# Layer 2's output projection in rounded passes, with casts and middle taps done by DMAs

## What is computed

```python
def _moe2_ref(x, w_in, conv_w, w_out):          # x: 4 x 1088 x 128
    h = np.maximum(x @ w_in, 0.0)               # 128 -> 1024 hidden channels
    conv_out = sum(conv_w[k] * hp[:, k:k + S, :] for k in range(3))   # hp is h, padded by one token
    gate = 1.0 / (1.0 + np.exp(-conv_out))
    return (h * gate @ w_out)                   # 1024 -> 128
```

## Time and profile before

| | |
|---|---|
| median of 3 runs | 256.98 us (256.5 to 289.55) |
| profiled execution, its own time | 256.51 us |
| its span, first to last instruction | 254.7 us |
| granted TensorE clock | 1.00 of full |
| instructions | 4283 |

### The profile page before, as it was taken

The page is one execution under the profiler, slowest core; times in us unless marked ns, Lnnn a source line. Parts: engine busy times, 40 slices in busy tenths (PEclk is TensorE's granted clock), DMA queues, the critical chain, the costliest instruction groups (busy, mean ns, idle before and its releaser), DMA issues.

```text
span 254.7 us, 4283 instructions
## 1 busy us (share of the span) xinstructions
PE 247.2 (97%) x1522; PEld 210.7 (83%) x1522; DVE 220.2 (86%) x404; ACT 157.0 (62%) x325; POOL 28.4 (11%) x90
## 2 busy tenths in 40 slices
PE   8999999999999999989999999999999999999995
PEld 7999999998989999978887777778778777777752
DVE  0847888899998688897799999999979999997992
ACT  2351733333586547688997766769769576667552
POOL 0000000001603343575200000000000000000000
PEclk9999999999999999999999999999999999999999
DMA  7959730300000000000000000002000002002002
GB/s 249 349 217 348 307 98 0 97 4 0 3 0 1 3 1 0 3 3 3 0 0 3 0 0 0 3 0 89 0 0 3 1 0 87 3 0 87 0 0 88
DMA packets 4340, 13.04 MB, mean 51 GB/s; under 512 B 736, under 2 KB 1504, under 8 KB 4320
## 3 DMA queue, kind: packets, MB, share of 16 engines
q1 hardware_dynamic: 4176, 12.74, 13.7%
q10 hardware_dynamic: 144, 0.03, 0.1%
HBM read 10.54 MB, written 2.23 MB: 50 GB/s over the span
## 4 chain that ended last, share of the span: by engine, by line
PE 46%; DVE 5%; ACT 3%; issue 2%; ACTq 0%
PE ps L600 20%; PE ps L521 7%; PE ps L523 7%; PE ps L522 7%; PE ps L561 5%; DVE arena L1061 2%; DVE arena L1056 1%; ACT arena L722 1%; ACT arena L798 1%; PE ps L552 1%; DVE arena L1068 1%; PE ps L531 0%; DVE x_nat L970 0%; DVE arena L977 0%; DVE x2lo L1004 0%
## 5 line engine op out<-in xcount | busy, mean ns | idle before, releaser
L600 PE MATMUL ps<-arena,wout 128*128 128x364 f32 (+1 forms) x192 | 62.8, 467 | 0.5 <-DVE arena L1068 0.5
L792 ACT ACTIVATE arena<-ps 128x364 f32<-128x364 f32 x96 | 42.6, 482 | 19.0 <-PE ps L523 16.8
L600 PEld LDWEIGHTS ps<-arena,wout 128*128 128x128 f32 x192 | 35.9, 189 | 20.6 <-issue 2.8
L1056 DVE SCALAR_TENSOR_TENSOR arena<-arena,ratio 128x1088 f32<-128x1088 f32 x32 | 43.1, 1346 | 1.9 <-ACT arena L792 1.9
L798 ACT ACTIVATE arena<-arena,base 128x1088 f32<-128x1088 f32 x32 | 38.8, 1211 | 7.3 <-DVE arena L1061 7.1
L1061 DVE SCALAR_TENSOR_TENSOR arena<-arena,ratio 128x1088 f32<-128x1088 f32 x32 | 43.1, 1346 | 0.1
L1068 DVE TENSOR_TENSOR arena<-arena 128x1088 f32<-128x1088 f32 (+2 forms) x36 | 41.3, 1159 | 1.5 <-ACT arena L798 1.3
L521 PE MATMUL ps<-x2hi,wlo 128*128 128x364 f32 x96 | 40.2, 419 | 0.7 <-ACT arena L736 0.4
L523 PE MATMUL ps<-x2hi,whi 128*128 128x364 f32 x96 | 31.5, 328 | 0.0
L522 PE MATMUL ps<-x2lo,whi 128*128 128x364 f32 x96 | 31.5, 328 | 0.0
L843 DVE TENSOR_TENSOR arena<-arena 109x1280 f32<-109x1280 f32 (+1 forms) x12 | 21.9, 1842 | 6.5 <-ACT arena L673 6.4
(11 more groups left out here) (100 smaller groups left out, 404.2 us busy)
## 6 DMA issues: line engine op xcount, KB each, us to landing
arena<-v_d SPq DMA_DIRECT2D x4, 594.0 KB, 3.9
arena<-qT_d SPq DMA_DIRECT2D x3, 545.0 KB, 5.9
arena<-kT_d SPq DMA_DIRECT2D x3, 544.5 KB, 5.0
out_d<-arena SPq DMA_DIRECT2D x3, 544.0 KB, 2.7
cos_t<-cos_d SPq DMA_DIRECT2D x1, 926.5 KB, 5.9
sin_t<-sin_d SPq DMA_DIRECT2D x1, 926.5 KB, 7.7
arena<-qT_d SPq DMA_DIRECT2D x2, 272.5 KB, 3.8
...
```

What stands on the lines that cost most here:

```text
L600: pe.matmul(ps[:, OUT_BANK + t, 0:z - a], wout[:, c, :], gate[:, i % GATES, a:z], start=(c == 0), stop=(c == C2 - 1)).then_inc(wout_done, 1)
L792: act.activation(h2[:, i % HIDDENS, t * TT:(t + 1) * TT], ps[:, bank_p(n), 0:TT], ACT.Relu).then_inc(h2_ready, 1)
L1056: dve.scalar_tensor_tensor(out=gate[:, i % GATES, :], in0=h2[:, i % HIDDENS, 0:S], scalar=ratio[:, 0, i % C2:i % C2 + 1], in1=h2[:, i % HI ...
```

## The change

- **Three rounded passes.** For the 14 chunks in `CAST` (1, 3, ... 27) `project` multiplies in three passes of rounded halves, as `hidden` does. GpSimd issues a DMA that casts the product to float32r (`cast_product`, high half), and VectorE subtracts that from the product (`product_low`, low half). `product_low(i)` stands in VectorE's iteration i + 4. `wout` gets halves too (`cast_wout`, `wout_low`), once.
- **Middle taps by DMA.** For the 18 chunks in `ADDED` (2, 4, ... 28 and 9, 15, 21, 25) VectorE's `left_tap` is left out. ScalarE copies `h2` times the left ratio to the gate's buffer (`left_copy`), a DMA of GpSimd's queue adds the middle tap from `h2` to it (`add_middle`), and `right_tap(i)` has moved to the start of VectorE's iteration i + 1.
- **Queues and buffers.** GpSimd's new loop has in iteration i `add_middle(i)`, then `cast_product(i - 2)`. There are 7 buffers for `gate`, given out by `gate_places`, and 3 pairs of halves; some tensors live in the rooms of earlier ones. `LAGS` is 6 throughout up to iteration 27, where it rose to 8 before.

```diff
-GATES = 9
+ADDED = tuple(sorted((*range(2, NI - 3, 2), 9, 15, 21, 25)))
+CAST = tuple(range(1, NI - 4, 2))
+CASTS, LOW_LAG = 3, 4
+H2_PAD, H2_ROW = 15, 1120
+GATES = 7
 SPLIT_FROM = NI - 2
-LAGS = ((-1, 6), (15, 7), (19, 8), (24, 7), (26, 6), (28, 5), (30, 4))
+LAGS = ((-1, 6), (28, 5), (30, 4))
...
+            def cast_wout():
+                pool.wait_ge(ld_wout, 32)
+                pool.wait_ge(whi_ready, 3)
+                pool.wait_ge(wlo_ready, 3)
+                pool.dma_start(wout_hi[:], wout.rearrange("p c d -> p (c d)")).then_inc(wout_hi_ready, 16)
...
+                if r == 4:
+                    cast_wout()
...
+            def add_middle(n, i):
+                pool.wait_ge(copied, n + 1)
+                if n >= 2:
+                    pool.wait_ge(middle_added[n % 2], 16 * (n // 2))
+                pool.dma_start(gate(i), h2(i)[:, 1:S + 1], accum_op=ALU.add).then_inc(middle_added[n % 2], 16)
+            def cast_product(n, i):
+                pool.wait_ge(prod_ready, i + 1)
+                if n >= 2:
+                    pool.wait_ge(cast_done[n % 2], 16 * (n // 2))
+                for free, count in halves_free(n):
+                    pool.wait_ge(free, count)
+                pool.dma_start(gate_hi[:, n % CASTS, :], gate(i)).then_inc(cast_done[n % 2], 16)
+            for i in range(NI):
+                if i in ADDED:
+                    add_middle(ADDED.index(i), i)
+                if i - 2 in CAST:
+                    cast_product(CAST.index(i - 2), i - 2)
...
+                n = CAST.index(i) if i in CAST else None
+                if n == 0:
+                    pe.wait_ge(wout_lo_ready, 1)
+                if i in CAST:
+                    pe.wait_ge(cast_done[n % 2], 16 * (n // 2 + 1))
+                    pe.wait_ge(low_ready, n + 1)
                 for t in range(NT):
-                    pe.wait_ge(prod_ready, products(i, t))
+                    if i not in CAST:
+                        pe.wait_ge(prod_ready, products(i, t))
                     if c == 0:
                         claim(OUT_BANK + t, (out_ready, 3 * b + t + 1))
                     a, z = t * TT, min((t + 1) * TT, S)
-                    pe.matmul(ps[:, OUT_BANK + t, 0:z - a], wout[:, c, :], gate[:, i % GATES, a:z],
+                    if i in CAST:
+                        w = slice(c * DM, (c + 1) * DM)
+                        three_pass(ps[:, OUT_BANK + t, 0:z - a], wout_hi[:, w], wout_lo[:, w], gate_hi[:, n % CASTS, a:z],
+                                   gate_lo[:, n % CASTS, a:z], c == 0, c == C2 - 1).then_inc(wout_done, 1)
+                        continue
...
+            def left_copy(i):
+                if i == ADDED[0]:
+                    act.wait_ge(ratios_ready, 2)
+                act.wait_ge(h2_ready, NT * (i + 1))
+                for free, count in gate_free(i):
+                    act.wait_ge(free, count)
+                act.activation(gate(i), h2(i)[:, 0:S], ACT.Copy,
+                               scale=ratio[:, 0, i % C2:i % C2 + 1]).then_inc(copied, 1)
...
+                    if i + 1 in ADDED:
+                        left_copy(i + 1)
...
             def left_tap(i):
                 dve.wait_ge(h2_ready, NT * (i + 1))
-                if i >= GATES:
-                    dve.wait_ge(wout_done, NT * (i - GATES + 1))
-                dve.scalar_tensor_tensor(out=gate[:, i % GATES, :], in0=h2[:, i % HIDDENS, 0:S], scalar=ratio[:, 0, i % C2:i % C2 + 1],
-                                         in1=h2[:, i % HIDDENS, 1:S + 1], op0=ALU.mult, op1=ALU.add).then_inc(left_ready, 1)
+                for free, count in gate_free(i):
+                    dve.wait_ge(free, count)
+                dve.scalar_tensor_tensor(out=gate(i), in0=h2(i)[:, 0:S], scalar=ratio[:, 0, i % C2:i % C2 + 1],
+                                         in1=h2(i)[:, 1:S + 1], op0=ALU.mult, op1=ALU.add).then_inc(left_ready, 1)
 
             def right_tap(i):
-                dve.wait_ge(left_ready, i + 1)
-                dve.scalar_tensor_tensor(out=gate[:, i % GATES, :], in0=h2[:, i % HIDDENS, 2:S + 2], scalar=ratio[:, 1, i % C2:i % C2 + 1],
-                                         in1=gate[:, i % GATES, :], op0=ALU.mult, op1=ALU.add).then_inc(conv_ready, 1)
+                if i in ADDED:
+                    n = ADDED.index(i)
+                    dve.wait_ge(middle_added[n % 2], 16 * (n // 2 + 1))
+                else:
+                    dve.wait_ge(left_ready, summed(i) + 1)
+                dve.scalar_tensor_tensor(out=gate(i), in0=h2(i)[:, 2:S + 2], scalar=ratio[:, 1, i % C2:i % C2 + 1],
+                                         in1=gate(i), op0=ALU.mult, op1=ALU.add).then_inc(conv_ready, 1)
 
             def product(i):
                 dve.wait_ge(gate_ready, i + 1)
                 cuts = [t * TT for t in range(NT)] if i >= SPLIT_FROM else [0]
                 for a, z in zip(cuts, cuts[1:] + [S]):
-                    dve.tensor_tensor(gate[:, i % GATES, a:z], h2[:, i % HIDDENS, 1 + a:1 + z], gate[:, i % GATES, a:z],
+                    dve.tensor_tensor(gate(i)[:, a:z], h2(i)[:, 1 + a:1 + z], gate(i)[:, a:z],
                                       ALU.mult).then_inc(prod_ready, 1)
+            def product_low(n, i):
+                dve.wait_ge(cast_done[n % 2], 16 * (n // 2 + 1))
+                for free, count in halves_free(n):
+                    dve.wait_ge(free, count)
+                dve.tensor_tensor(gate_lo[:, n % CASTS, :], gate(i), gate_hi[:, n % CASTS, :].bitcast(F32),
+                                  ALU.subtract).then_inc(low_ready, 1)
+            def wout_low():
+                dve.wait_ge(wout_hi_ready, 16)
+                dve.tensor_tensor(wout_lo[:], wout.rearrange("p c d -> p (c d)"), wout_hi[:].bitcast(F32),
+                                  ALU.subtract).then_inc(wout_lo_ready, 1)
...
-                if i < NI:
+                if i - 1 in ADDED:
+                    right_tap(i - 1)
+                if i < NI and i not in ADDED:
                     left_tap(i)
                 if i + 1 in LAST_TURNS:
                     normed_low(LAST_TURNS[i + 1])
@@ -1082,8 +1198,12 @@
                     slot(n)
                 if i >= 2:
                     product(i - 2)
-                if i < NI:
+                if i < NI and i not in ADDED:
                     right_tap(i)
+                if i == 3:
+                    wout_low()
+                if i - LOW_LAG in CAST:
+                    product_low(CAST.index(i - LOW_LAG), i - LOW_LAG)
...
+def gate_places():
+    places, until = [], [-1] * GATES
+    for i in range(NI):
+        place = min(range(GATES), key=lambda n: until[n])
+        places.append(place)
+        until[place] = i + LOW_LAG if i in CAST else next(n for n in range(NI + FINAL_LAG) if n + 1 - lag(n) > i)
+    return places
```

More of the change, by code:

```diff
@@ L50 @@
 AB = 2 * R
-ARENA = 19612
+ARENA = 12720
 PADS = 4
@@ L189, in build @@
         h1 = room(128, 3, G1)
-        h2 = room(128, HIDDENS, SP)
-        gate = room(128, GATES, S)
+        h2_homes = [x_room[:, n * H2_ROW:(n + 1) * H2_ROW] for n in range(2)] + [room(128, H2_ROW) for _ in range(HIDDENS - 2)]
+        gate_homes = [folded_room[:, n * S:(n + 1) * S] for n in range(2)] + [room(128, S) for _ in range(GATES - 2)]
         outT = room(128, S)
@@ L277, in products, with summed, h2, gate @@
             return i + 1 if i < SPLIT_FROM else SPLIT_FROM + NT * (i - SPLIT_FROM) + t + 1
+        def summed(i):
+            return i - sum(n < i for n in ADDED)
+        def h2(i):
+            return h2_homes[i % HIDDENS][:, H2_PAD:H2_PAD + SP]
+        def gate(i):
+            return gate_homes[GATE_OF[i]]
+        def gate_free(i):
+            last = max((n for n in range(i) if GATE_OF[n] == GATE_OF[i]), default=None)
+            if last is None:
+                return ()
+            return ((low_ready, CAST.index(last) + 1),) if last in CAST else ((wout_done, NT * (last + 1)),)
+        def halves_free(n):
+            return ((wout_done, NT * (CAST[n - CASTS] + 1)),) if n >= CASTS else ()
         def written(unit):
@@ L771, in _ @@
                     act.wait_ge(ld_w, 48)
-                    for a, z in ((0, D1), (D1, 2 * D1), (2 * D1, 2 * D1 + D2)):
+                    for a, z in ((0, D1), (D1, 2 * D1)):
                         act.activation(whi[:, a:z], wraw[:, a:z], ACT.Copy).then_inc(whi_ready, 1)
+                    act.activation(whi[:, 2 * D1:], win_raw[:], ACT.Copy).then_inc(whi_ready, 1)
             feature_copies(B - 1)
```

52 lines of the change are left out of this document (34 added, 18 removed).

## The result

The changed kernel takes 303.5 us (median of 6 runs, 302.62 to 335.15) against 256.78 for the kernel before on the same chip (6 runs, 256.46 to 289.55). The ratio is 1.182, with a 95% interval of 1.179 to 1.185: slower by 47 us. I had forecast 267 and a range of 257 to 283. Some executions are disturbed and about 30 us or more longer (those of 335.15 and 289.55 us, for example): ratios, and the times of the experiments, leave them out, and of experiments 7, 8 and 12 only such a one was profiled.

The account below looks back on a forecast made before the run. TensorE bounds layer 2, VectorE 2 us behind. After the change the GpSimd loop's waits decide: body +2.0, product_low(25) +1.2, end +1.6 and +5.8, together +10.6 on 256.5, so 267 us; range 257 to 283.

Parts of the forecast that it names:

- The loop through GpSimd: GpSimd's in-order queue: an add waits behind a cast for an odd product, delaying right_tap; body +2.0 us.
- 4.8 us of relief: TensorE: 14 projections in three passes save 0.34 us each, 4.8 us, hidden in the sum because TensorE waits for VectorE.
- VectorE's account: VectorE: 18 left taps go (22.7 us), 14 low halves and one of wout come; net 4.6 us less.
- ScalarE's: ScalarE's account: 18 copies at 1.1 us, 20 us in all, fit into its idle time; nothing charged.
- L: Time from the end of an odd product to the landing of the add, against 3.7 us of VectorE cover.
- I take 4.6: Choice of 4.6 us for L, cast and add DMAs in a row, priced from the store's row; 13 waits.
- My own wider bracket, from loads: Upper bound on L from load DMAs of this size: two less one fixed part, 6.3 to 8.5 us.
- the prediction's sum: Body from product(1) to right_tap(28): 13 waits L, 12 tap-and-product stretches, less left taps, plus slots; 101.6 us at L = 4.6.
- Rival C: Slow DMAs, L from 5.2 to 7, perhaps GpSimd held up beside VectorE, giving 284 to 301 us; chance 0.18.
- case B: Loop covered, L at most 3.9; TensorE bounds the body, idles 8.4 us for last low halves; 260 us, chance 0.28.
- +5.8 and +2.8: End: project(27) waits for product_low(27), then two projections remain, +5.8 us; +2.8 from right_tap(28) to the end of product(29).
- "Start: 0": Start, up to product(1): same taps and products for chunks 0 and 1, wout's cast in idle GpSimd; 0 us.

Follow-up runs that it names:

- experiment 7: Changed kernel, but TensorE runs 24 passes with unused results ahead of projections 23, 25 and 27: 295.3 us, ratio 1.150.
- experiment 8: Changed kernel without casts, so adds alone, with nine gate buffers and the lags of the kernel before: 258.5 us, ratio 1.006.
- experiment 12: Lag 7, eight gate buffers and cast behind add, with high halves copied by a GpSimd instruction instead of the casting DMA: 281.7 us, ratio 1.096.
- experiment 3: Changed kernel without casts: all projections in float32, the 18 adds by DMA stay: 259.1 us, ratio 1.011.
- experiment 2: Changed kernel with a plain copy DMA in place of the accumulating add, so the left tap is missing from the result: 290.2 us, ratio 1.131.
- experiment 6: Changed kernel with the cast issued behind the add, projections up to 26 one chunk later (lag 7), and eight gate buffers: 278.4 us, ratio 1.084.
- experiment 1: Changed kernel with only GpSimd's order altered, the add issued ahead of the cast: 291.4 us, ratio 1.136.
- experiment 5: Changed kernel without the last three casts (chunks 23, 25 and 27), which go to the float32 projection: 283.2 us, ratio 1.103.

## Why the prediction was wrong

**The direction and the place were right.** The loop through GpSimd is there, eleven of the thirteen rounds have a `right_tap` that waits for a DMA, TensorE waits for VectorE, and no 4.8 us of relief appear. VectorE's account (net 4.6 less; measured 3.6 less busy) and ScalarE's (the copies fit: experiment 3 has TensorE without a gap) hold.

**The step that failed first: "I take 4.6, since source and destination here are SBUF and the store ... is the nearest row".** L was 6.3. The cast did land as such a store would (3.0, have 2.7); the add did not. It moves its bytes at 186 GB/s, 3.0 us alone, where I had allowed 1.2 to 2.4, and 5.4 us pass to its landing when the cast runs beside it. My own wider bracket, from loads, began at 6.3. That accumulation alone makes the difference is shown by experiment 2, where the plain copy brings L to 4.7. An operation that no row shows (an addition in flight) should have been priced from that side, or left as wide as it was; at 1.3 us per 0.1 of L, 1.7 of L are 22 us. The edge at L = 5.8 left out the measured value. With 6.3 in its place the prediction's sum gives 289, so this step is 22 of the 36 us that were missing, and the next ones are the rest.

**Rival C came nearest, with the wrong mechanism.** Its 284 to 301 came from L = 5.9 to 7.2, and the measured L lies in that, but it got there through GpSimd being held up beside VectorE; that it came within 3 us of 303.5 is luck, since it lacked the waits of TensorE too. In the changed kernel GpSimd's issues took 0.54 to 0.56 us for a cast and 0.86 to 0.96 for an add, beside a VectorE at work (161.10 us: 0.91) and an idle one (164.33 us: 0.88) alike. By the rule of the Trainium skill that the prediction cited (SBUF — State Buffer, SBUF: two separate sides) a DMA's issue isn't held, and these rows agree. The other page of the Trainium skill (DMA: Bandwidth & Descriptors, Anatomy of one DMA — SWDGE (gpsimd) path) gives such a DMA 2.0 us and its bytes over 436 GB/s, an estimate of 3.3; the cast's 3.0 and the plain copy's 3.0 agree, the add's 4.8 alone on the engines doesn't.

**The step that was missing: TensorE's side of the low halves.** I let `project` wait in the body for nothing. But at lag 6 the projection of a cast chunk needs product, cast, low half in time, and behind the waiting projection stands the `hidden` from which the next copies and adds come. Experiment 2 shows that the step was missing: with L at 4.7 the body was still 17 us longer than the sum. Experiment 6 shows its size: the order of the queue gave 12 us (experiment 1), one chunk of lag with its buffer 13 more. The two loops share the waits, so neither has a price of its own in the 31.8 us of the body; the split "22 by L" is what one loop alone would cost.

**The end was +5.8 and +2.8 in the forecast, +8.4 and +5.6 in the trace.** The order-bound waits were there (5.37, 4.20, 5.71 us of idle TensorE against the 0.7, 2.2 and 5.5 of case B, so the first two were too short as well), and I priced what follows them at full clock. Experiment 7 gives 8.2 us for keeping the clock up; some of it may be in the body, since projection 23 stands ahead of `right_tap(28)`. The wait of `sigmoid(26)` behind `output(2)` was not in my order of the end at all; a copy that is executed once in eight chunks is easily read past. All late casts together are worth 20.3 us (experiment 5).

**"Start: 0"** was +1.3. No experiment looks at it, so the cause stays open.

So the 47 us: the three late casts 20 (14 at the end, 5 in the body); most of the rest in two loops, which tighter order and one chunk of lag bring from a body of 131.4 us to one of 106.0 with all casts in place (experiment 6; before 99.65); and 2 to 3 that the adds cost by themselves (experiments 3 and 8). These parts overlap. No version tried beats the kernel before. None could by much: TensorE had no gap, adds don't relieve it, and 14 projections in three passes relieve it by 4.8 us at best.
